# Block 1's mixing taps summed by TensorE in plain f32, with its mixing weights loaded ahead of layer 2's w_in

## What is computed

```python
w = softmax(weight_gen)                      # 8 heads, 7 taps per token
x = einsum('bshk,bskhg->bshg', w, x_unf)     # each token mixes itself and the 6 before it
h = x @ w_in1                                # 192 -> 2048
g = (a0 + a1*h + a2*h2 + a3*h3) / (1 + |b0||h| + |b1|h2 + 1e-6)
x = g @ w_out1                               # 2048 -> 192
h = x @ w_in2
g = h * clip(h + 3, 0, 6) / 6
y = g @ w_out2
```

## Time and profile before

| | |
|---|---|
| median of 3 runs | 1242.54 us |
| the profiled execution | 1243.18 us |
| its span, first to last instruction | 1241.4 us |
| mean granted TensorE clock | 0.995 of full |
| TensorE matmul, VectorE, ScalarE, GpSimd busy | 96%, 94%, 94%, 91% |

### The profile page before, as it was taken

How to read it: one execution, slowest core, us unless ns; L and a number is a source line. 1 busy time by engine, 2 the same in 40 slices (tenths; PEclk the granted TensorE clock), 3 DMA queues, 4 the chain that set the end, 5 groups by cost and what they waited for, 6 DMA issues and landing times.

```text
span 1241.4 us, 19302 instructions
## 1 busy us (share of the span) xinstructions
PE 1197.4 (96%) x5211; PEld 975.5 (79%) x5211; DVE 1170.6 (94%) x1884; ACT 1169.6 (94%) x2197; POOL 1133.7 (91%) x892
## 2 busy tenths in 40 slices
PE   6676999999999999999999999999999999999998
PEld 5444788888888888888888888888888888888876
DVE  8899999999999999999999999999999999999933
ACT  6888999999999999999999999999999999999954
POOL 7999899999999999999999999999999999966664
PEclk9989999999999999999999999999999999999999
DMA  8863132233313233321322333122333212010000
GB/s 202 170 148 64 42 77 52 60 73 81 68 42 75 55 75 73 73 60 40 89 58 60 73 79 68 39 70 64 68 73 73 60 48 47 14 22 22 5 22 18
DMA packets 64774, 80.79 MB, mean 65 GB/s; under 512 B 15832, under 2 KB 42200, under 8 KB 64408
## 3 DMA queue, kind: packets, MB, share of 16 engines
q1 hardware_dynamic: 63464, 77.59, 27.1%
q0 software_dynamic: 1200, 1.97, 1.4%
HBM read 57.49 MB, written 9.98 MB: 54 GB/s over the span
## 4 chain that ended last, share of the span: by engine, by line
PE 90%; DVE 4%; ACT 2%; issue 2%; DMA 1%; POOL 1%; DVEq 0%; SPq 0%; ACTq 0%
PE h L750 9%; PE acc L757 9%; PE acc L767 9%; PE acc L764 9%; PE acc L761 9%; PE acc L758 9%; PE h L751 9%; PE h L752 9%; PE h L753 9%; PE h L754 9%; DMA late<-in_moe_w_in 1%; DVE early L1261 1%; DVE early L1255 1%; PE h L774 1%; DVE q_recip L1269 1%
## 5 line engine op out<-in xcount | busy, mean ns | idle before, releaser
L683 POOL TENSOR_TENSOR g_lo<-late,g_hi 128x512 fp32r<-128x512 f32 x255 | 344.2, 1350 | 60.8 <-ACT g_hi L1034 40.6
L673 POOL TENSOR_TENSOR g_lo<-early,g_hi 128x512 fp32r<-128x512 f32 x256 | 345.5, 1350 | 1.7 <-ACT g_hi L1011 1.6
L750 PE MATMUL h<-x_hi,w_in_hi 128*128 128x512 f32 x511 | 202.7, 397 | 21.6 <-DVE early L1285 20.7
L1293 DVE SCALAR_TENSOR_TENSOR late<-late,h 128x512 f32<-128x512 f32 x256 | 174.3, 681 | 42.1 <-ACT late L1022 40.6
L764 PE MATMUL acc<-g_lo,w_out 128*128 128x512 f32 x512 | 200.4, 391 | 1.7 <-POOL g_lo L673 1.7
L757 PE MATMUL acc<-g_hi,w_out 128*128 128x512 f32 x512 | 199.7, 390 | 0.8 <-DVE x_lo L1299 0.7
L767 PE MATMUL acc<-g_lo,w_out 128*128 128x512 f32 x512 | 200.0, 391 | 0.0
L761 PE MATMUL acc<-g_hi,w_out 128*128 128x512 f32 x512 | 199.9, 390 | 0.0
L758 PE MATMUL acc<-g_hi,w_out 128*128 128x512 f32 x512 | 199.8, 390 | 0.0
L751 PE MATMUL h<-x_lo,w_in_hi 128*128 128x512 f32 x511 | 199.5, 390 | 0.0
L752 PE MATMUL h<-x_hi,w_in_lo 128*128 128x512 f32 x511 | 199.3, 390 | 0.0
(11 more groups left out here) (115 smaller groups left out, 2414.0 us busy)
## 6 DMA issues: line engine op xcount, KB each, us to landing
mix_w<-mix_weights SPq DMA_DIRECT2D x75, 192.0 KB
mix_w<-mix_weights SPq DMA_DIRECT2D x75, 144.0 KB
x_win<-in_x SPq DMA_DIRECT2D x15, 393.0 KB, 3.2
mix_w<-mix_weights SPq DMA_DIRECT2D x60, 96.0 KB
mix_w<-mix_weights SPq DMA_DIRECT2D x60, 72.0 KB
late<-late SPq DMA_DIRECT2D x32, 128.0 KB, 2.3
out_y<-late SPq DMA_DIRECT2D x16, 256.0 KB, 2.0
x_tail_hi<-tail_hi SPq DMA_DIRECT2D x60, 64.0 KB, 2.0
```

Source lines behind the costliest of these rows:

```text
L673: nc.gpsimd.tensor_tensor(g1_lo[p][:, :], neg_g[p], g1_hi[p][:, :].bitcast(F32), ALU.subtract).then_inc(g1_lo_ready, 1)
L683: nc.gpsimd.tensor_tensor(g2_lo[p][:, :], gate[p], g2_hi[p][:, :].bitcast(F32), ALU.subtract).then_inc(g2_lo_ready, 1)
L750: pe.matmul(out[:, :], w_hi[:, cols], hi[:, :], start=True, stop=False)
```

## The change

For block 1 alone, GpSimd no longer adds. It writes its products by turns into the two halves of `mix`, and TensorE sums them in PSUM with a matmul by the identity in plain f32 (not float32r), in two banks that layer 2's sums use later: 512 columns into acc2[0], 256 into acc2[1]. ScalarE rounds from PSUM. VectorE takes the rests from PSUM at step 13, in place of GpSimd at steps 14 and 15. The copies by `copy_hi` use the same banks, so the first two of them now wait for that. The softmax weights of part 1 are scaled at step 3 instead of 5, and stored and loaded back before w_in2 is loaded. The rounding of w_in2, of its tail and most of w_out2 moves to later steps. The table of part 2's softmax steps (THIRD_EARLY, the maximum at step 19 among them) stays as it is. Blocks from 2 on are mixed as before.

```diff
+        tap_sum = [acc2[0], acc2[1][:, 0:HALF]]
...
-        PRODUCT_STEPS_1 = {5: (0, 1,), 6: (2,), 7: (3,), 8: (4,), 10: (5,), 12: (6,)}
-        ADD_STEPS_1 = {6: (1,), 7: (2,), 8: (3,), 9: (4,), 11: (5,), 13: (6,)}
+        PRODUCT_STEPS_1 = {5: (0, 1,), 6: (2,), 7: (3,), 8: (4,), 9: (5,), 10: (6,)}
+        ADD_STEPS_1 = {6: (0, 1,), 7: (2,), 8: (3,), 9: (4,), 10: (5,), 11: (6,)}
+        SECOND_LO = 13
...
-        IN_HI = {6: ((1, 0),), 7: ((1, 1),), 8: ((1, 2), (1, 3),)}
-        TAIL_HI = {7: ((1, 0),), 8: ((1, 1),), 9: ((1, 2),), 10: ((1, 3),)}
-        OUT_HI = {1: ((0, 0),), 3: ((0, 1),), 5: ((0, 2),), 7: ((0, 3),), 9: ((1, 0),), 10: ((1, 1),), 11: ((1, 2),), 16: ((1, 3),)}
-        OUT_LO = {2: ((0, 0),), 6: ((0, 1),), 7: ((0, 2),), 10: ((0, 3),), 13: ((1, 0), (1, 1),), 16: ((1, 2),), 19: ((1, 3),)}
-        EXP_1, SUM_1, RECIP_1, SCALE_1 = 1, 1, 2, 5
+        IN_HI = {14: ((1, 0),), 16: ((1, 1),), 17: ((1, 2),), 18: ((1, 3),)}
+        TAIL_HI = {13: ((1, 0),), 14: ((1, 1),), 15: ((1, 2),), 16: ((1, 3),)}
+        OUT_HI = {1: ((0, 0),), 3: ((0, 1),), 5: ((0, 2),), 7: ((0, 3),), 13: ((1, 0),), 14: ((1, 1),), 17: ((1, 2),), 18: ((1, 3),)}
+        OUT_LO = {2: ((0, 0),), 6: ((0, 1),), 7: ((0, 2),), 10: ((0, 3),), 15: ((1, 0),), 17: ((1, 1),), 19: ((1, 2),), 21: ((1, 3),)}
+        EXP_1, SUM_1, RECIP_1, SCALE_1 = 1, 1, 2, 3
...
-            load_tail(1, w_in2, slice(0, F), in2_tail_staged)
-            sp.wait_ge(in1_lo, 4)
-            sp.dma_start(in_slot, w_in2[0:P, :]).then_inc(in2_staged, 16)
             sp.wait_ge(gen_scaled, 2)
             store_gen(1)
             sp.wait_ge(gen_stored[1], 16)
             load_mix_w(1, slice(A_TAPS, K), mix_w_b)
+            load_tail(1, w_in2, slice(0, F), in2_tail_staged)
+            sp.wait_ge(in1_lo, 4)
+            sp.dma_start(in_slot, w_in2[0:P, :]).then_inc(in2_staged, 16)
...
+                if blk == 1:
+                    if k > 1:
+                        pool.wait_ge(taps_taken, k - 1)
+                    out = mix[:, k % 2, :]
...
+                def take_taps(c):
+                    if s == -1:
+                        for k in ADD_STEPS_1.get(c, ()):
+                            pe.wait_ge(mix_product_ready, k + 1)
+                            pe.matmul(tap_sum[0], ident_r[:, :].bitcast(F32), mix[:, k % 2, 0:BLOCK], start=k == 0,
+                                      stop=k == K - 1)
+                            pe.matmul(tap_sum[1], ident_r[:, :].bitcast(F32), mix[:, k % 2, BLOCK:MIX], start=k == 0,
+                                      stop=k == K - 1).then_inc(taps_taken, 1)
...
                         if n + COPY_LAG == (s + 1) * NC + c:
+                            if j < 2:
+                                pe.wait_ge(x1_hi_ready, 1)
+                                pe.wait_ge(x1_tail_hi_ready, 1)
+                                pe.wait_ge(x1_second_lo, 1)
+                                pe.wait_ge(x1_second_tail_lo, 1)
...
                     layer2_out(c)
+                    take_taps(c)
                     copy_hi(c)
...
+                    if n == SECOND_LO:
+                        dve.wait_ge(x1_tail_hi_ready, 1)
+                        dve.tensor_tensor(tail_lo[:, :], tap_sum[1], tail_hi[:, :].bitcast(F32),
+                                          ALU.subtract).then_inc(x1_second_tail_lo, 1)
+                        dve.wait_ge(x1_hi_ready, 1)
+                        dve.tensor_tensor(x1[1][1][:, :], tap_sum[0], x1[1][0][:, :].bitcast(F32),
+                                          ALU.subtract).then_inc(x1_second_lo, 1)
```

More of the change, by code:

```diff
@@ L202, in build_program @@
         hi_copied = sem("hi_copied")
+        taps_taken = sem("taps_taken")
         acc1_added = sem("acc1_added")
@@ L233, in build_program @@
         x1_first_lo = sem("x1_first_lo")
+        x1_second_lo = sem("x1_second_lo")
+        x1_second_tail_lo = sem("x1_second_tail_lo")
         gen_max = sem("gen_max")
@@ L490, in copy_tail @@
                                      tail_hi[half * D2:(half + 1) * D2, :].bitcast(F32)).then_inc(tail_hi_copied, 16)
-                sp.wait_ge(x1_tail_lo_ready, count(1, blk, 0))
+                if blk == 1:
+                    sp.wait_ge(x1_second_tail_lo, 1)
+                else:
+                    sp.wait_ge(x1_tail_lo_ready, count(1, blk, -1))
                 for rows in (0, D2):
@@ L631, in mix_product @@
                     pool.wait_ge(mix_w_a, count(16 * MIX_DMAS, blk, 0))
-                    if blk > 1:
+                    if blk == 2:
+                        pool.wait_ge(taps_taken, K)
+                    if blk > 2:
                         pool.wait_ge(x1_hi_ready, count(1, blk, -1))
                         pool.wait_ge(x1_tail_hi_ready, count(1, blk, -1))
-                        pool.wait_ge(x1_lo_ready, count(1, blk, -1))
-                        pool.wait_ge(x1_tail_lo_ready, count(1, blk, -1))
+                        pool.wait_ge(x1_lo_ready, count(1, blk, -2))
+                        pool.wait_ge(x1_tail_lo_ready, count(1, blk, -2))
                 if k == A_TAPS:
                     pool.wait_ge(mix_w_b, count(16 * MIX_DMAS, blk, 0))
[L640 to L644, removed]
+                if blk == 1:
+                    if k > 1:
+                        pool.wait_ge(taps_taken, k - 1)
+                    out = mix[:, k % 2, :]
+                else:
+                    if k == 1 and blk > 2:
+                        pool.wait_ge(mix_added, count(K - 1, blk - 3, K - 1))
+                    if k > 1:
+                        pool.wait_ge(mix_added, count(K - 1, blk - 2, k - 1))
+                    out = mix_sum if k == 0 else mix_part
                 nc.gpsimd.tensor_tensor(
@@ L687, in mixing @@
                     if is_block(s + 2):
-                        for k in add_steps(s).get(c, ()):
-                            mix_add(s + 2, k)
+                        if s > -1:
+                            for k in add_steps(s).get(c, ()):
+                                mix_add(s + 2, k)
                         for k in product_steps(s).get(c, ()):
                             mix_product(s + 2, k)
-                        if c == X1_TAIL_LO:
+                        if c == X1_TAIL_LO and s > -1:
                             split_x1_tail_lo(s + 2)
-                        if c == X1_LO:
+                        if c == X1_LO and s > -1:
                             split_x1_lo(s + 2)
@@ L805, in layer1_in @@
                             pe.wait_ge(x1_hi_ready, count(1, s, 1))
-                            pe.wait_ge(x1_lo_ready, count(1, s, 1))
+                            if s == 0:
+                                pe.wait_ge(x1_second_lo, 1)
+                            else:
+                                pe.wait_ge(x1_lo_ready, count(1, s, 0))
                             pe.wait_ge(tail_hi_copied, count(64, s, 64))
@@ L961, in round_x1_tail @@
             def round_x1_tail(blk):
-                act.wait_ge(mix_added, count(K - 1, blk - 1, K - 1))
-                if blk > 1:
+                if blk == 1:
+                    act.wait_ge(taps_taken, K)
+                else:
+                    act.wait_ge(mix_added, count(K - 1, blk - 2, K - 1))
                     act.wait_ge(tail_hi_copied, count(64, blk - 2, 64))
-                act.copy(tail_hi[:, :], mix_sum[:, BLOCK:MIX]).then_inc(x1_tail_hi_ready, 1)
+                act.copy(tail_hi[:, :], tap_sum[1] if blk == 1 else mix_sum[:, BLOCK:MIX]).then_inc(x1_tail_hi_ready, 1)
             def round_x1(blk):
-                act.wait_ge(mix_added, count(K - 1, blk - 1, K - 1))
-                act.copy(x1[blk % 2][0][:, :], mix_sum[:, 0:BLOCK]).then_inc(x1_hi_ready, 1)
+                if blk == 1:
+                    act.wait_ge(taps_taken, K)
+                else:
+                    act.wait_ge(mix_added, count(K - 1, blk - 2, K - 1))
+                act.copy(x1[blk % 2][0][:, :], tap_sum[0] if blk == 1 else mix_sum[:, 0:BLOCK]).then_inc(x1_hi_ready, 1)
             def segment(s):
```

## The result

The changed kernel is slower: 1247.55 us, median of 8 runs (1246.64 to 1248.24), against 1242.89 for the kernel before in the same runs (median of 8). The ratio is 1.0031, with a 95% interval of 1.0023 to 1.0040. The profiled execution took 1247.59 us, its span is 1245.5.

The account below looks back on a forecast made before the run. Before 140 us VectorE's steps set the pace, so step 20's start decides; afterwards TensorE is always busy. Terms −8.0 + 6.25 + 3.35 + 0.2 = +1.8 took the median from 1242.54 to 1244.3 us; range 1240.2 to 1247.2.

Parts of the forecast that it names:

- front gain: Steps 6 to 12: step 13 begins at 73.65 us instead of 81.66, a gain of 8.0 us.
- GpSimd, steps 3 to 8: Walk through GpSimd's instructions with its additions removed: step 7 begins at 49.2 us, step 8 at 54.0.
- The seven taps: TensorE's identity matmuls for block 1, 768 columns each: 1.36 us per tap, hidden in idle time, cost nothing.
- The queue of SyncE: Part 1's store goes out at 31.6 us, taps 4 to 6 land by 44, w_in2 loads end near 55: hidden.
- Steps 13 to 18: Seven moved splits, x1's rests and a new wait make these steps 30.3 us; step 19 begins at 103.95.
- The coupling at the copy: Step 14: TensorE's copy waits for VectorE's rests of x1, holding acc matmuls and ScalarE's roundings; 1.1 us.
- Step 19: Eighth split (0.66 us), then VectorE's maximum stalls 2.7 us for part 2's load; the step takes 8.0 us.
- The clock: Falls of TensorE's clock after idling before step 14's copy and in step 19's stall: 0.2 us, bounds 0 to 0.9.
- The swap: Slower rival, chance 0.22: layer 1's tail-sum swap queues behind part 2's load, delaying GpSimd from step 21; 1 to 2.5 us.
- Taps at the low clock: Slower rival: clock falls in steps 7 to 11, about 1.3 us each, 1246 to 1247; chance 0.12 including a slow load landing.
- Faster: Rival, chance 0.16: front gain larger or kept, end at 1241.5 us, or 1238.8 if part 2's load were hidden too.
- the gain of the reordered loads: Step 6: ScalarE no longer waits for w_in2, which helps by 3.56 us.

Follow-up runs that it names:

- the three repairs: Changed kernel with part 2's first maximum at step 20, SyncE's swap ahead of the load and TensorE's acc matmuls before step 14's copy: 1242.49 us, ratio 0.9994.

## Why the prediction was right where it was, and where it was not

The mechanism was right: a front gain of 8.0 (measured 7.93), most of it forecast to go in steps 13 to 18 (6.25; measured 8.04) and the rest and more in step 19 (3.35; measured 3.61). The sign of the sum was right too, +1.8 forecast. The size was too small: by the ratio the median moved by 3.9 us (0.31% of 1242.89), over the 0.2% bound, where I had 0.55 on "within" and 0.32 on "slower". The range ended at 1247.2. The ratio puts the forecast's starting point, 1242.54, at 1246.4, inside it; the median itself, 1247.55, is above it, as the kernel before was 0.35 us longer in these runs as well.

- *GpSimd, steps 3 to 8.* Right to 0.1 us at steps 7, 8 and 13. The walk along the busiest engine, start by start, gave this; no busy share would have. It says that two additions go up to L673 of step 7; the timeline of before has one there (42.37), and the sum doesn't use the count.
- *The seven taps.* Hidden, as said. From the first L914 to the second acc matmul of step 9 (59.17 to 60.69, less one matmul of 0.23) a tap takes 1.29; I had 1.36, from L774, whose instructions are transposes; that they came so near is in part luck.
- *The queue of SyncE.* Right: the store went out at 31.61, taps 4 to 6 were issued from 38.12, w_in2 at 44.14, and nobody waited for any.
- *Steps 13 to 18.* 32.08 against 30.3. VectorE's share was right: a step with one split takes 4.61 where nothing else holds it. The coupling at the copy was priced at 1.1, with ScalarE's four roundings in it; both together are 1.2 (0.8 and 0.46). It came with 1.3 of low clock, and step 16 had another 0.5.
- *Step 19.* 8.24 against 8.0, the stall 2.94 against 2.7. With the maximum moved, step 19 lasts 4.96, so this is shown. The fit that the prediction takes from the Trainium skill ("DMA: Bandwidth & Descriptors") stands there for DMAs that GpSimd issues; this load is SyncE's, and the trace agrees all the same, with 2.5 from issue to landing for the six loads of 224 KB.
- *The clock.* This is the term that was sized too small: "I take 0.2 for them, between 0 and two falls of 0.45". Measured, it is 1.3 in step 14, about 0.5 in step 16 (perhaps by chance) and 0.4 in step 20: 2.2 in all, 2.0 more than the term. With 0.2 from the stall and 0.1 at step 13 this is the missing part at step 24 (130.2 forecast, 132.54 measured). I had taken the price of a fall from a step where the matmuls had slack. In step 14 they stood behind a wait that had used the slack up: the copy and the five acc matmuls, which ScalarE waits for, came at 0.43 instead of 0.23 us, and these six lay on the path whole. With TensorE kept busy in the wait, that 1.3 went. Of the two places that I had named for a fall, the copy of step 14 was right. The one that cost step 20 its 0.4 began ahead of the stall of step 19, and came without it too. The rule of the Trainium skill ("TensorE: Matmul & The Clock Gate", HAM oscillation), that TensorE falls back to the low clock where it waits for DMAs between bursts of matmuls, pointed to more loss at steps 19 to 21 than my term. The trace of the changed kernel doesn't bear it out there: the clock falls at 108.1 us, and the wait for the DMA begins at 110.26; it only stays at 0.50 through the wait, until 118.

The rivals. The swap was real but hidden in the changed kernel: the stall beside it was longer. It showed at once when the stall went, 2.3 us, near the upper end of the 1 to 2.5 that I had given it. Taps at the low clock did not come: between 40 and 77 us the clock is full. Faster was refuted by steps 13 to 18 and by step 19. The prediction puts the gain of the reordered loads at the 3.56 of step 6; the run without the taps has 0.83 there, and it moves the splits too, so what the order of the loads is worth by itself isn't shown.

What stays open: why a low stretch comes at step 18 in one execution and at step 16 in another, though the programs are the same up to there. The runs show where it fell, and after what idleness, but I did not make an experiment that forecasts it, and each kernel's steps are read from one execution.

## What to carry to other kernels

When work is taken off an engine, ask which later steps get the work that moved, and give the free time of the relieved engine to them. Here GpSimd stood idle for 10.8 us between 65 and 82 us. With four splits put there, and TensorE's order in step 14 changed, the kernel is 0.3% faster instead of 0.3% slower; the new order alone gave 0.1%. For each piece that is moved later, look for who waits for the last one of its kind: here a load, a maximum and a swap stood behind "all eight splits", and their waits lay beside each other. The trace of the changed kernel shows both the stall of 2.94 us and GpSimd's wait of 4.0; what each costs came out only when the other was taken away. Price a fall of the clock by the slack of the step in which it lands, not by what another step lost.

## What the runs showed that I had not expected

A plain f32 matmul of 128 x 128 by 512 columns is issued as two instructions (14 L914 for seven taps), and a tap of 768 columns takes 1.29 us, 3.8 times the 0.34 of float32r matmuls at 0.227 per 512 columns. In a wait of 3.0 us of TensorE the clock fell to half, and it stayed there to 84 us, 6 us behind the wait; this cost 1.3 us of the 1247, and eleven useless matmuls removed it. The same fall came in the kernel with the three repairs and cost nothing, as no engine on the path waited for the matmuls in it.
